# Gated linear recurrence and two gated feed-forward layers: the work around the attention halves is put into another order

## What is computed

```python
def _attn_ref(q, k, v, i_gate, f_gate, o_gate):      # B, H, S, D = 2, 8, 768, 40
    for t in range(S):
        m_new = np.maximum(f_gate[:, :, t] + m, i_gate[:, :, t])
        f_stab = np.exp(f_gate[:, :, t] + m - m_new)
        i_stab = np.exp(i_gate[:, :, t] - m_new)
        m = m_new
        C = f_stab * C + i_stab * einsum('bhd,bhe->bhde', v_t, k_t)
        n = f_stab * n + i_stab * k_t
        denom = np.maximum(np.abs(n . q_t), 1.0)
        y[:, :, t] = sigmoid(o_gate_t) * (C q_t) / denom
# x: (1536 tokens, 320)
xn = x / sqrt(mean(x * x) + 1e-06) * rms_g
x2 = (silu(xn @ w_gate) * (xn @ w_val)) @ w_out             # 320 -> 1536 -> 320
out = (sigmoid(x2 @ w2_gate) * (x2 @ w2_val)) @ w2_out      # 320 -> 1536 -> 320
```

## Time and profile before

| | |
|---|---|
| median of 3 runs | 537.88 us |
| the profiled execution | 540.02 us |
| its span in the profile | 538.2 us |
| mean granted TensorE clock | 0.948 |
| TensorE busy (matmuls / weight loads) | 507.9 us (94%) / 421.6 us (78%) |
| VectorE, ScalarE, GpSimd busy | 246.6, 215.4, 100.2 us |
| chain that ended last | PE 76%, POOL 6%, ACT 6%, issue 5%, DVE 4%, DMA 2% |

### The profile page before, as it was taken

One profiled execution on the slowest core, in us unless ns is written; L12 is line 12 of the kernel. 1 busy time (PEld: TensorE's weight loads), 2 busy tenths in 40 slices (PEclk: granted clock), 3 DMA queues, 4 the chain that ended last, 5 costly groups with the idle time before them and its releaser, 6 DMA issues.

```text
span 538.2 us, 7463 instructions
## 1 busy us (share of the span) xinstructions
PE 507.9 (94%) x2660; PEld 421.6 (78%) x2660; DVE 246.6 (46%) x503; ACT 215.4 (40%) x444; POOL 100.2 (19%) x108
## 2 busy tenths in 40 slices
PE   0898998989999999999999999999999999999996
PEld 0486887878777888888888999888888888888884
DVE  5866567678565454452323665422223222322222
ACT  3455567666565533252322555422222222222122
POOL 4335376677534300000000000000000000000000
PEclk9756599879899999999999999999999999999999
DMA  6746656763534100001012143000001000010001
GB/s 147 198 112 174 161 154 165 201 178 84 154 79 108 58 1 1 1 12 38 24 38 71 31 148 119 0 2 0 0 1 49 1 0 1 0 49 0 0 0 49
DMA packets 18145, 35.14 MB, mean 65 GB/s; under 512 B 2320, under 2 KB 10992, under 8 KB 18112
## 3 DMA queue, kind: packets, MB, share of 16 engines
q1 hardware_dynamic: 17824, 34.38, 23.4%
q10 hardware_dynamic: 288, 0.33, 0.3%
HBM read 31.46 MB, written 2.16 MB: 62 GB/s over the span
## 4 chain that ended last, share of the span: by engine, by line
PE 76%; POOL 6%; ACT 6%; issue 5%; DVE 4%; DMA 2%; SPq 0%; ACTq 0%; DVEq 0%; POOLq 0%
PE bank L1035 47%; PE bank L1050 6%; PE bank L1051 6%; PE bank L1052 5%; PE bank L1059 3%; PE bank L1058 3%; PE bank L994 2%; POOL wo_split L408 2%; POOL q_st L375 1%; POOL k_st L382 1%; PE bank L983 1%; PE bank L962 1%; DMA rhs_rows<-gate_rows 1%; PE bank L1000 1%; DVE gv_split L789 1%
## 5 line engine op out<-in xcount | busy, mean ns | idle before, releaser
L1035 PE MATMUL bank<-x_hi,gv_split 128*128 128x512 f32 (+2 forms) x840 | 254.5, 373 | 0.3 <-ACT hid L521 0.3
L1035 PE MATMUL bank<-x_lo,gv_split 128*128 128x512 f32 (+2 forms) x504 | 183.8, 369 | 0.0
L1035 PEld LDWEIGHTS bank<-x_hi,gv_split 128*128 128x128 f32 x840 | 156.4, 195 | 26.7 <-ACT hid L521 0.5
L1035 PEld LDWEIGHTS bank<-x_lo,gv_split 128*128 128x128 f32 x504 | 98.3, 195 | 15.5
L821 DVE TENSOR_TENSOR hid<-hid,bank 128x512 f32<-128x512 f32 (+1 forms) x60 | 38.0, 633 | 151.9 <-PE bank L1035 151.7
L528 ACT ACTIVATE hid_hi<-hid 128x512 fp32r<-128x512 f32 (+1 forms) x84 | 48.0, 571 | 143.1 <-DVE hid L821 106.1
L521 ACT ACTIVATE hid<-bank 128x512 f32<-128x512 f32 (+1 forms) x84 | 44.6, 531 | 119.6 <-PE bank L1035 119.6
L828 DVE TENSOR_TENSOR hid_lo<-hid,hid_hi 128x512 fp32r<-128x512 f32 (+1 forms) x84 | 54.2, 646 | 42.9 <-ACT hid_hi L528 42.9
L1050 PE MATMUL bank<-hid_hi,wo_split 128*128 128x512 f32 (+1 forms) x168 | 61.1, 364 | 0.3 <-DVE hid_lo L828 0.3
L1051 PE MATMUL bank<-hid_lo,wo_split 128*128 128x512 f32 (+1 forms) x168 | 61.1, 364 | 0.0
L1052 PE MATMUL bank<-hid_hi,wo_split 128*128 128x512 f32 (+1 forms) x168 | 60.5, 360 | 0.0
(11 more groups left out here) (112 smaller groups left out, 501.6 us busy)
## 6 DMA issues: line engine op xcount, KB each, us to landing
qk_raw<-qk SPq DMA_DIRECT2D x24, 480.0 KB, 4.6
gv_raw<-wgv SPq DMA_DIRECT2D x24, 384.0 KB, 3.1
wo_raw<-wo SPq DMA_DIRECT2D x24, 160.0 KB, 2.7
v_sb<-v SPq DMA_DIRECT2D x12, 168.0 KB, 4.5
gate<-og SPq DMA_DIRECT2D x12, 160.0 KB, 4.6
k_sb<-k SPq DMA_DIRECT2D x10, 160.0 KB, 4.4
outT<-y_out SPq DMA_DIRECT2D x6, 256.0 KB, 2.0
s_st<-s_st SPq DMA_DIRECT2D x10, 52.5 KB
```

Source lines behind the costliest of these rows:

```text
L1035: mm = pe.matmul(ps[:, 0:size], lhs, rhs, start=(i == 0), stop=(i == len(passes) - 1))
```

## The change

The tables of blocks and slots are replaced by a list of units, `UNIT_LIST`. The first layer now has three blocks of 512 tokens. In the first of them the feature groups 0 to 6 are done in two units of 256 columns each (first all seven for tokens 0 to 255, then all seven for tokens 256 to 511) and the groups 7 to 11 in units of 512. That makes 79 units: 14 of 256 columns and 65 of 512. The last two blocks are written out, there is no hardware loop.

`FIRST` = 4: the prelude holds the halves 0 to 3 and not 0 to 4. `HALF_AT` puts the halves 4 to 23 and what follows them into the units 0 to 7, 9, 11, 13 to 21, 23, 25, 26 and 27; `PREP_AT` puts the weight steps 2 to 11 into the units 0 to 4, 8, 10, 12, 14 and 15.

The prelude is written out by hand for every engine. Its scores are plain fp32 products of the q and k as loaded (40 rows), so rounding and stacking of q and k is left out for the halves 0 to 3. The first part of the gate rows is one chunk wide instead of two (128 and 640 columns instead of 256 and 512). The constant rows are written by GpSimd and ScalarE instead of VectorE, the small row operands have four buffers instead of two, an exponential is run early on ScalarE, the mask has its own transfer, and the products that keep TensorE at work are 8, 2, 2, 2, 8 and 8 instead of 10 and 8.

In a unit with a half, TensorE takes the gate products first, then `exponents`, `outputs`, `state_sums`, value products, `scores`, results and `turn_x`. `exponents` and `scores` share bank 5 from half 4 on.

```diff
-LEAD = 5
 HALVES = 2 * NT
+FIRST = 4
 LOG_STEP = (5, 4)
 DECAY_AT = 2 * CH * B * H
-BLOCKS = [(0, 0, 256), (0, 256, 512), (0, 768, 512), (0, 1280, 256),
-          (1, 0, 512), (1, 512, 512), (1, 1024, 512)]
-B0, B1 = 4, len(BLOCKS)
-UNITS = B1 * NF
-TANH_UNITS = 2 * NF
-C_IDENT, C_MASK, C_ALPHA = 0, P, P + HG * L
+SPLIT = 7
+UNIT_LIST = ([(0, 0, f, 0, 256) for f in range(SPLIT)] + [(0, 0, f, 256, 256) for f in range(SPLIT)]
+             + [(0, 0, f, 0, TB) for f in range(SPLIT, NF)]
+             + [(b // 3, b, f, TB * (b % 3), TB) for b in range(1, 6) for f in range(NF)])
+UNITS = len(UNIT_LIST)
+ENDS = [max(u for u in range(UNITS) if UNIT_LIST[u][1] == b) + 1 for b in range(6)]
+B0, B1 = 3, 6
+PART1 = ENDS[B0 - 1]
+LAST_BLOCK = ENDS[B0 - 2]
+TANH_UNITS = ENDS[1]
+HALF_AT = dict(zip([0, 1, 2, 3, 4, 5, 6, 7, 9, 11, 13, 14, 15, 16, 17, 18, 19, 20, 21, 23, 25, 26, 27],
+                   range(FIRST, HALVES + 3)))
+PREP_AT = dict(zip([0, 1, 2, 3, 4, 8, 10, 12, 14, 15], range(2, NF)))
...
-CONST_ROWS = 4
-PARTS = [(0, 2), (2, CH)]
+C_MASK = C_END
...
+TURNS = {2 * t + 4: t for t in range(2, NT)}
+SCALES = {2 * t + 3: t for t in range(2, NT)}
+WARM_START, WARM_SLOT, WARM_TURN = 8, 2, 8
...
+        early = lambda tile: tile[0:D].rearrange("p (h s) -> p h s", h=HG)
+        qk_early = [(early(hid[0]), early(hid[1])), (early(swap), early(y_tail))]
...
-        arg_ps = lambda j: bank[j % 2] if before(j) else bank[5]
-        s_ps = lambda j: bank[2 + j % 2] if before(j) else bank[3] if own_bank(j) else bank[5]
-        pv_ps = lambda j: bank[6]
+        arg_ps = lambda j: bank[j % 2] if j < FIRST else bank[5]
+        s_ps = lambda j: bank[2 + j % 2] if j < FIRST else bank[5]
+        pv_ps = bank[6]
         st_ps = bank[7]
-        xt_ps = lambda t: bank[4] if before(turn_slot(t)) else bank[7]
...
+            for j in range(FIRST):
                 load_qk(j)
             load_v(0)
             load_gate(0)
             load_k(0)
             store_rows(0)
...
+            load_v(1)
+            load_gate(1)
+            for n in range(2):
+                load_gv(n)
+                load_wo(n)
+            for j in range(FIRST, FIRST + 2):
+                load_qk(j)
+            store_rows(1)
+            load_k(1)
+            load_v(2)
+            load_gate(2)
+            sp.wait_ge(rows_out, 16 * 2)
+            for j in range(FIRST, FIRST + 2):
+                load_rows(j)
+            spread_state(0)
+            for u in range(-1, PART1 + 1):
...
             less_m(0)
             pool.wait_ge(consts_in, 16)
+            for i in range(4):
+                nc.gpsimd.tensor_copy(rhs_rows[i][0:2 * HG], sel_rows(consts)).then_inc(rows_const, 1)
             pool.wait_ge(gains_in, 16)
             nc.gpsimd.tensor_tensor(gain_tail[:], gain_col[:, 2:3], alpha_w, ALU.mult).then_inc(gain_done, 1)
-            stack(0)
-            stack(1)
...
+            pool.wait_ge(cols_done, 1)
+            weigh_v(0)
+            rest_logs()
+            root(0)
+            weigh_v(1)
+            root(1)
+            rest_wo(0)
+            stack(FIRST)
+            rest_wo(1)
...
-            act.dma_start(consts[:], const).then_inc(consts_in, 16)
+            act.dma_start(consts[:], const[:, 0:C_END]).then_inc(consts_in, 16)
+            act.dma_start(mask_raw, const[:, C_MASK:]).then_inc(mask_in, 16)
             act.dma_start(gain_col[:], gains).then_inc(gains_in, 16)
+            act.wait_ge(setup_pool, 4)
+            nc.scalar.activation(act_warm[:], half_pow[:], ACT.Exp)
             act.wait_ge(consts_in, 16)
+            nc.scalar.activation(ident_bf[:], ident, ACT.Copy).then_inc(const_act, 1)
+            act.wait_ge(mask_in, 16)
+            nc.scalar.activation(mask_bf[:], mask_raw, ACT.Copy).then_inc(const_act, 1)
...
+            gate_tanh(0)
+            exponential(0)
+            round_rows(1)
+            exponential(1)
+            gate_exponentials(1)
+            gate_tanh(1)
+            exponential(2)
+            exponential(3)
+            round_gv(0)
+            sum_squares(0)
+            round_qk(FIRST)
+            scale_y(0)
+            round_wo(0)
+            sum_squares(1)
+            round_state(0)
+            round_x(0)
+            scale_y(1)
+            round_x(1)
+            round_gv(1)
+            round_wo(1)
+            for u in range(UNITS):
+                slot = HALF_AT.get(u, -1)
+                t, g = slot // 2, slot % 2
+                activate(u)
+                if u in HALF_AT:
+                    if slot < HALVES:
+                        exponential(slot)
+                    if slot in SCALES:
+                        sum_squares(SCALES[slot])
+                    if slot + 1 < HALVES:
+                        round_qk(slot + 1)
+                    if g == 0 and t <= NT - B:
+                        round_state(t - 1)
+                round_hidden(u)
                 if slot in SCALES:
...
-            for g in range(2):
-                nc.vector.tensor_scalar(lhs_rows[g][:], consts[0:LR_ROWS, 0:L], 0.0, 1.0, ALU.mult,
-                                        ALU.add).then_inc(const_dve, 1)
-                nc.vector.tensor_copy(rhs_rows[g][0:2 * HG], sel_rows(consts)).then_inc(const_dve, 1)
-            nc.vector.tensor_copy(ident_bf[:], ident).then_inc(const_dve, 1)
-            nc.vector.tensor_copy(mask_bf[:], consts[:, C_MASK:C_MASK + HG * L]).then_inc(const_dve, 1)
-            rest_rows(0)
-            stack_k(0)
+            rest_rows()
+            weight_rows(0)
             gate_logs(1)
+            weight_rows(1)
             take_columns(0)
...
             def exponents(j):
-                g = j % 2
-                pe.wait_ge(rows_in[g], 32 * (j // 2 + 1))
-                if before(j):
+                i = j % 4
+                pe.wait_ge(rows_in[i], 32 * (j // 4 + 1))
+                if j < FIRST:
                     need(pe, exp_done, j - 1)
-                elif own_bank(j - 1) or own_bank(j):
-                    pe.wait_ge(exp_done, j)
                 else:
                     pe.wait_ge(p_done, j)
...
             def scores(j):
                 g = j % 2
-                pe.wait_ge(q_stacked, j + 1)
-                pe.wait_ge(k_stacked, j + 1)
-                if before(j):
+                if j < FIRST:
+                    q_raw, k_raw = qk_early[g] if j >= 2 else (qk_raw[g][0:D, 0], qk_raw[g][0:D, 1])
+                    if j < 2:
+                        pe.wait_ge(qk_in[g], 16 * qk_loads(j))
+                    else:
+                        pe.wait_ge(early_in[g], 32)
                     need(pe, p_done, j - 1)
-                elif own_bank(j):
-                    pe.wait_ge(p_done, j)
-                else:
-                    pe.wait_ge(exp_done, j + 1)
+                    for h in range(HG):
+                        mm = pe.matmul(s_ps(j)[:, L * h:L * h + L], k_raw[:, h], q_raw[:, h], start=True, stop=True)
+                    mm.then_inc(s_done, 1)
+                    return
+                pe.wait_ge(q_stacked, j + 1 - FIRST)
...
+            pe.wait_ge(const_act, 2)
+            turn_gates(0)
+            keep_clock_up(WARM_START)
+            pe.wait_ge(rows_const, 8)
+            exponents(0)
+            scores(0)
+            exponents(1)
+            scores(1)
+            keep_clock_up(WARM_SLOT)
+            outputs(0)
+            exponents(2)
+            scores(2)
+            keep_clock_up(WARM_SLOT)
+            outputs(1)
+            exponents(3)
+            scores(3)
+            state_sums(0)
+            keep_clock_up(WARM_SLOT)
+            outputs(2)
+            turn_gates(1)
+            pe.wait_ge(diag_done, 1)
+            pe.matmul(bank[4][0:D, DECAY_AT:DECAY_AT + NT * H], ones[:], c_diag[:].rearrange("p c b h -> p (c b h)"),
+                      start=True, stop=True).then_inc(cols_ps, 1)
+            outputs(3)
+            keep_clock_up(WARM_TURN)
+            pe.wait_ge(cols_done, 3)
+            turn_x(0)
+            keep_clock_up(WARM_TURN)
+            turn_x(1)
+            for u in range(UNITS):
+                slot = HALF_AT.get(u, -1)
...
+                gate_products(u)
+                if 0 <= slot < HALVES:
+                    exponents(slot)
+                if FIRST < slot <= HALVES:
+                    outputs(slot - 1)
+                if u in HALF_AT and g == 0 and t <= NT - B:
+                    state_sums(t - 1)
+                value_products(u)
+                if 0 <= slot < HALVES:
+                    scores(slot)
+                if u > 0:
+                    result_products(u - 1)
+                if slot in TURNS:
                     turn_x(TURNS[slot])
```

550 lines of the change are left out of this document (224 added, 326 removed).

## The result

| | before | after |
|---|---|---|
| median (4 runs each) | 537.89 us | 545.0 us (543.39 to 547.79) |
| ratio to before, 95% interval | | 1.014 [1.009, 1.019] |
| profiled execution, span | 540.02, 538.2 us | 547.79, 546.0 us |
| U (start of the first slot with a unit) | 46.4 us | 47.2 us |
| TensorE idle from U to 220 us | 7.6 us | 10.9 us |

What follows compares the result with a forecast made beforehand. The prediction took the kernel from 332 us on as pure TensorE time, with waits and lowered clock before 157 us. 41.9 + 463.9 + 12.3 + 6.5 = 524.6 us span, plus 1.8, less 2.1: 524.3 us; range 516 to 534.

Steps and rivals of the forecast that it cites:

- U: Prelude, up to the start of the first slot with a unit: from 46.4 to 41.9 us.
- W: TensorE's work at full clock behind the prelude: 463.9 us, 1.3 more than before.
- S: Everything lost behind the prelude, waits and clock: 12.3 us, where it was 22.7.
- E: The tail of the span, after the last unit's results: 6.5 us.
- the clock, sized at 2.0: Behind the prelude: clock rises about when units start, TensorE having no long wait after; 2.0 us lost, where 9.7 were.
- heavy slots: Units 0 to 4, each with a half and a weight step: 5 x 1.56 = 7.8 us lost.
- -3.0: Prelude's gate rows: VectorE's first product with scores comes 3.0 us earlier.
- -2.1 - 3.7 - 4.1 + 2.6: Prelude, us: `rhs_rows` wait gone; half 4 moved out; no rounding and stacking of q and k; fp32 scores.
- A: Rival: the 30 clock products keep TensorE at 2.4 GHz throughout; 518.9 us, chance 0.19.
- B: Rival: idle time between the two transpositions drops the clock for 19.45 us as units start; 528.9 us, chance 0.14.
- C: Rival: the prelude is no shorter, 46.4 us; total 528.8 us, chance 0.15.
- D: Rival: exponents and scores sharing bank 5 make 20 halves wait 1.0 us each; 544.3 us, chance 0.10.

Runs made afterwards that it cites:

- e16: Kernel before with GpSimd's root ahead of its operations on state and v: 530.78 us, 0.987 of the kernel before.
- e2: Changed kernel with eight clock products ahead of unit 7's and of unit 13's gate products: 543.35 us, 1.013 of the kernel before.
- e3: Changed kernel with GpSimd's root ahead of its operations on state and v: 536.47 us, 0.999 of the kernel before.
- e4: Changed kernel with the first block split over eight feature blocks instead of seven, the eighth's weights readied in unit 5: 552.36 us, 1.031.
- e9: Changed kernel with the gate column copies ahead of half 3, first transposition right behind its products with v, ten clock products between transpositions: 542.59 us, 1.011.
- e10: Changed kernel with GpSimd's root first, split over eight, no clock products between halves, gate columns and first transposition early: 529.85 us, 0.988.
- e18: Changed kernel with GpSimd's root first, halves in units 0 to 22, first block split over eight feature blocks: 532.56 us, 0.991.
- e7: Changed kernel with the halves in units 0 to 22, one in each, instead of spread over units 0 to 27: 540.95 us, 1.010.
- e17: Changed kernel with GpSimd's root first and the halves in units 0 to 22, one in each: 536.48 us, 1.000.
- e1: Changed kernel with only the eight clock products at the start, the other 22 left out: 544.5 us, 1.015.
- e5: Changed kernel without the six clock products between its first four halves, the sixteen around the transpositions kept: 542.77 us, 1.012.
- e8: Changed kernel with the load of q and k ahead of the weights in SyncE's queue: 544.6 us, 1.017.
- e14: Changed kernel, root first, split over eight, none between halves, columns and first transposition early, q and k first, twelve clock products at start: 528.98 us, 0.982.

## Why the prediction was wrong

The forecast had U 41.9, W 463.9, S 12.3 and E 6.5. After has U 47.2, E 6.5 (value products end at 537.6, a third of a unit later 539.5, span 546.0), and if W is as worked out, S = 546.0 - 47.2 - 463.9 - 6.5 = 28.4. The miss is 5.3 in U and 16.1 in S.

**S: the clock, sized at 2.0, was 18.7.** This is the step that failed: "TensorE has no long wait after that". The three falls of 10.24 us above cost 15.4, and the two of 3.4 us behind U 1.7 each. The rest of S was right as a sum, in part by luck: heavy slots 7.8, unit 7 1.5 and others 1.0 make 10.3, and TensorE's idle times over 0.3 us behind U sum to 10.1. Of these 4.7 lie in the units 0 to 4; unit 7's was 2.43, near the upper end named for it; and unit 13's 2.53 was in no term, as from unit 8 on no wait above 0.5 us was expected. The forecast's own list held a wait of up to 2.65 us and five slots with 1.56 us each, and gave none of them a fall of the clock. The kernel before had shown such falls: its clock of 0.90 from 65.88 to 118.66 was taken for part of the 1.56 us a slot, where e16 showed that moving one GpSimd instruction takes the falls away and leaves the idle time. The two kernels lose nearly the same clock behind U, 17.4 and 19.0 us: of the long fall as the units start (45.42 to 65.90, 9.7 us of clock behind U) the change left 1.7, as forecast, and in place of 6.8 us in three later falls it has 17.1 in four.

The Trainium skill, "TensorE: Matmul & The Clock Gate", part 1, says that idle time brings the throttle back; e2 agrees, with the clock at 1.00 where the idle time was filled. It also says that sustained work releases it; the 23.63 us of unbroken work at 0.51 in the prelude do not agree, as the earlier trace rows did not. The same part warns that the records of the throttle can be unreliable. e2 bears this out:

```profile
14.32:38.00 23.68, 23.35 (x103) 18.45 (x103) 6.62 (x18) 9.36 (x20) 5.03 (x5) 1.00 0.48 133
```

```profile
14.32 2.07 PE L975 MATMUL bank<-qk_raw 40*128 40x128 f32 x8
16.33 0.79 PE L960 MATMUL bank<-rhs_rows,lhs_rows 10*128 10x512 f32 x1
```

The granted clock reads 1.00, but the four products take 16.33 - 14.32 = 2.01 us, the pace that they have at half clock. e3, e4, e9, e10 and e18 have this too, up to about 41 us; behind U the clock as read agrees with the sum of the spans above. The distance between equal instructions is the clock to trust.

**The spread was priced at a gain.** That "a unit with a half alone or a weight step alone leaves GpSimd 2.6 or 1.75 us to do" was not the fault. What I left out is the other side: a unit without a half gives TensorE only 2.85 us of work behind a slot whose ScalarE work is late. e7 puts this at 4.0 us, of which e17 leaves nothing once the root is early.

**U: one term had no ground.** In three parts, before and after: start of the first exponents, 17.67 and 12.96; from there to the eight clock products ahead of a transposition (40.15 and 36.52), 22.5 and 23.6; from there to U, 6.3 and 10.7. The forecast's terms in the same parts: -3.0; -2.1 - 3.7 - 4.1 + 2.6 and half of the clock products' 3.8, -5.4; the other half and the transpositions' 2.0, +3.9. The start was better than forecast (-4.7; VectorE's first product with scores stands at 15.18, promised at 16.6), the end as forecast (+4.4). The middle was to shrink by 5.4 us and grew by 1.1. Windows of the kernel before, finer than the earlier trace rows, show why:

```profile
24.19:42.94 18.75, 18.66 (x95) 14.30 (x95) 12.02 (x29) 8.67 (x21) 5.51 (x7) 0.52 0.57 142
```

TensorE was busy there at half clock already; 20.00 to 46.43 as one stretch had mixed this with the waits at either end. So rounding and stacking of q and k were hidden behind TensorE, and the -4.1 for them is 0 by these rows; no run leaves out this step alone. Four fp32r scores at half clock took 27.90 - 26.87 = 1.03 us before:

```profile
26.87 1.09 PE L983 MATMUL bank<-q_st,k_st 120*128 120x128 f32 x4
27.90 0.60 PE L943 MATMUL bank<-consts,w_row 16*128 16x16 f32 x4
```

The fp32 scores, which were to cost +0.65 a half, cost 2.00 - 1.03 = 0.97 at half clock and 1.08 - 0.56 = 0.52 at full, 3.4 us for the four (one of them at full clock) instead of 2.6. The twelve more clock products, priced at 3.8, cost no more than the 3.3 that e1 gave for leaving out 22, of which the six between the halves are 2.4 (e5), all to the 2 us that a U is good for. With -4.1 at 0, the scores at 3.4 and the six products at 2.4 the middle comes out at 0 instead of -5.4; the last 1.1 us stay open.

The wait for `rhs_rows` of 2.06 us went, as forecast, and 1.11 us of it came back ahead of the first exponents. The page of the Trainium skill that the prediction cited for the gate rows, "SBUF — State Buffer", section on who interferes with whom, was right about one instruction:

```profile
8.98 0.81 DVE L664 TENSOR_TENSOR keep_log<-fi_row,m_row 16x640 f32<-16x640 f32 x1
9.03 2.17 POOL L373 TENSOR_TENSOR fi_row<-fi_row,m_row 16x640 f32<-16x640 f32 x1
...
9.83 2.04 DVE L668 TENSOR_TENSOR keep_log<-keep_log,m_row 16x640 f32<-16x640 f32 x1
```

Two VectorE operations of one shape take 0.81 and 2.04 us; the second ends 0.67 us after GpSimd's. It cost 1.2 us beside TensorE's chain, and not the 2.6 that the rule was given.

**Right**: W and the unit's 5.58 us, E, the weights of the second layer and the written-out blocks at 0 (TensorE is busy for all 205.00 us from 332 on), the 10.3 of waits as a sum. **The rivals**: A did not come. B's condition did not: no fall lasts from the first unit for 19 us, though its mechanism, idle time and a fall behind it, is the one that decided, at other places. C (U as long as before, 528.8) was right on U and says nothing of S. D, the only one on the slower side, is refuted: line 960 waited once for VectorE's product, 0.4 us, where it needed 1.0 in each of 20 halves. The kernel became slower by falls at places that no rival had. Of what would show the forecast wrong, both came: U above 46, and TensorE standing for more than 6 us.

## What to carry to other kernels

Price a wait of TensorE with the fall of the clock behind it. Behind U, in the traces of all twenty kernels, each of the 32 waits of 1.4 us and more came with a fall, which began between 0.8 us before its end and 2.3 us behind; at the waits of 2.1 to 3.3 us the falls lasted 6.8 to 13.7 us and so cost 3.4 to 6.8. Of 43 waits between 1.0 and 1.3 us at full clock only ten came with one. Work taken from a crowded slot is also taken from the cover behind it; before thinning slots out, follow each engine's queue to see what stands behind an instruction that waits, as one early root was worth 1.3 to 1.5% in both kernels. And before an operation on another engine is counted as saved, look at the shortest stretch around it for whether TensorE is busy there.

## What the runs showed of the hardware

- Behind U the clock falls for 3.4, 6.8, 10.2 or 13.7 us at a time (17.1 once, in e8), with TensorE busy nearly throughout; three falls of the changed kernel last 10.24 us each. After waits of 1.0 to 1.3 us it fell in some places (behind 121.17 us in e10 and 118.04 in e14) and not in others.
- A profile's granted clock can read 1.00 over 23.68 us in which the pace is that of half clock.
- Four fp32 products of 40 by 128 by 128 take 1.08 us at full clock and 2.00 at half; four fp32r products of 120 by 128 by 128 take 1.03 at half.
- The prelude's clock is at half from about 13 to 18 us on by execution, filled start or not, with TensorE at work since 8 us, and stays there to about 40. U of one prelude differs by up to 4 us between executions.
